# A linear-attention pair whose states go from VectorE to ScalarE, with products read from PSUM and masks over two banks

## The chip, the cores and the metric

The kernel runs on one core of one Trainium2 chip. The metric is device time of one execution in microseconds (us). The trace is one execution taken by the hardware profiler. Engines: PE is TensorE (PEld its weight loads), DVE is VectorE, ACT is ScalarE, POOL is GpSimd, SP is SyncE (it only starts transfers here).

## What is computed

Three stages follow each other. The change touches the first alone.

```python
# B, H, S, D = 4, 8, 768, 48
for t in range(S):                      # per batch and head
    cur = outer(u * k[t], v[t])
    y[t] = r[t] @ (state + cur)
    state = w[t][:, None] * state + outer(k[t], v[t])
# then, on the 3072 tokens x 384 of y: a mixture of 8 experts (top 1), and
# out = max(x @ m1, x @ m2, x @ m3) @ mo
```

## The kernel before, in words

**Tiling.** Two heads of one batch are a pair; each head takes 64 of the 128 partitions, 48 of them used, the features of the head. There are ALL = 16 pairs, n = 0 to 15. The 768 steps are six chunks (CH) of 128; a half (HALF) is three chunks. One PSUM bank holds 512 float32 per partition, so a half of a pair (3 x 128) fits in one bank and a pair needs two.

**One pair, by data.** PE turns the raw w, k and r (tokens on partitions) to features on partitions, a half at a time (`turn_raw`, L1397): w and k into banks 0 and 1, r into banks 2 and 3. ACT copies each half to SBUF (`take`, L652): `decay`, `k_t`, `r_t`. DVE scans the decays backward (`suffix_of`, L947) and forward (`prefix_of`, L959), both with a running product over 774 elements, into `products`, and multiplies them into the keys (`keys_of`, L970) and the receptances (`receptance_of`, L979). PE makes scores of 128 x 128 within each chunk from both, one half at a time (`scores`, L1412), into banks 2 and 3 (one bank per head). DVE copies the scores over a prepared tile `score` under a triangular mask, one instruction for each bank (`mask`, L995). That tile was written by POOL with the diagonal (`own_diagonal`, L580), from `own`, which DVE sums (`own_of`, L988) out of POOL's two products of raw r, raw k and u (`own_products`, `own_times_u`, L557 to L570). For what goes from chunk to chunk PE turns the weighted keys (`keys`, L1426), ACT copies them out (`key_rows_of`, L684), PE makes a 48 x 48 sum for each of the first five chunks (`key_values`, L1435) into bank 6, DVE carries them from chunk to chunk in a scan (`carry`, L1005) that is written back to bank 6, and scales them by the decays at the chunk borders into `state` (L1017), five matrices. PE adds values times scores (`mix_values`, L1451) and states times receptances (`mix_state`, L1470), ACT copies the result out (`columns`, L691), PE turns it to rows of tokens (`rows_of`, L1481), and ACT copies these and stores them to DRAM from its own queue (`tokens_of`, L698). One more pass of ACT reads all 1548 products of the pair to find whether any has grown out of range (`spread_of`, L677); `suffix_of` of the pair after next waits for it, since it writes the same buffer.

**Order.** Every engine runs one instruction stream in order, written out by hand. All per-pair buffers are double (index n % 2), except the banks. In round n:

- DVE: mask(n,0), own_of(n+1), mask(n,1), prefix_of(n+1), carry(n) with the states, on some rounds small sums for the routing (n = 4, 8, 12 and 5, 9, 13), keys_of(n+1), receptance_of(n+1), suffix_of(n+2).
- PE: scores(n,0), keys(n), turn k of n+1, scores(n,1), turn w of n+2, rows_of(n-1,1), turn r of n+1, key_values(n), mix_values(n,0 and 1), mix_state(n,0 and 1), rows_of(n,0).
- ACT: key_rows_of(n), take k of n+1, take w of n+2, tokens_of(n-1,1), take r of n+1, spread_of(n), columns(n,0 and 1), total_of(n+1), tokens_of(n,0). (`total_of`, L669, spreads the decays of the chunk borders for `carry`.)
- POOL: waits for suffix_of(n+1), then own_products(n+2), own_times_u(n+2), own_diagonal(n+1).
- SP: loads w, k, r and v of pair n+4 when the buffers come free.

Before the rounds, DVE works out unit embeddings of the experts, and in round 0 it fills `to_rows`, the matrix that `rows_of` multiplies by (`rows_matrix`, L934).

Of the kernel before, what the change touches and what calls it, by code (L numbers as in the profile page):

```python
# [5 lines left out]
ALU = mybir.AluOpType  # L6
ACT = mybir.ActivationFunctionType
AX = mybir.AxisListType.X
F32 = mybir.dt.float32
# [6 lines left out]
def linear_attention_moe_max_mlp(nc, r, k, v, w, u, emb, tau, w1, w2, m1, m2, m3, mo, out):  # L16
# [102 lines left out]
    k_t = sb("k_t", [P, 2, CH, P])  # L119
    r_t = sb("r_t", [P, 2, CH, P])  # L120
# [113 lines left out]
    with ctx:  # L234
        bank = [ctx.enter_context(nc.psum_tensor(f"bank{i}", [P, 512], F32)) for i in range(8)]
# [28 lines left out]
        x_stored = [sem(f"x_stored{i}") for i in range(XR)]  # L264
        emb_sq, emb_root, emb_unit, emb_turned, emb_ready = (
# [263 lines left out]
        def _(pool):  # L529
# [61 lines left out]

            pool.wait_ge(suffix_ok, 2)
            own_products(0)
# [50 lines left out]
        def _(act):  # L644
# [7 lines left out]
            def take(n, name):  # L652
                if name == "w" and n >= 2:
                    act.wait_ge(prefix_ok, n - 1)
                if name == "k" and n >= 2:
                    act.wait_ge(key_ok, n - 1)
                if name == "r" and n >= 2:
                    act.wait_ge(rec_ok, n - 1)
                if n == 0:
                    act.wait_ge(decay_set, 2)  # L660
                for x in range(2):
                    act.wait_ge(turned, turn_no(n, name, x) + 1)
                    src = bank[x + (2 if name == "r" else 0)][:, 0:HALF * P].rearrange("q (c t) -> q c t", c=HALF)
                    half = slice(HALF * x, HALF * (x + 1))
                    dst = (k_t if name == "k" else r_t)[:, n % 2, half] if name != "w" else \
                        decay[:, n % 2, 1:].rearrange("q (c t) -> q c t", c=CH)[:, half, 0:P]
                    act.copy(dst, src).then_inc(taken, 1)

            def total_of(n):  # L669
                act.wait_ge(suffix_ok, n + 1)  # L670
                if n >= 2:
                    act.wait_ge(state_ready, n - 1)
# [11 lines left out]
            def key_rows_of(n):  # L684
# [4 lines left out]
                act.copy(key_rows[:, 4, :], bank[6][:, 256:256 + P]).then_inc(rows_taken, 1)  # L689

# [32 lines left out]
            take(0, "w")  # L723
            take(0, "k")
            act.wait_ge(zeroed, 4)
            take(0, "r")
            total_of(0)
            take(1, "w")
# [165 lines left out]
        def _(dve):  # L894
# [19 lines left out]
            mark(dve.memset(to_rows[:, :, :], 0.0))  # L914
# [19 lines left out]
            def rows_matrix():  # L934
                dve.wait_ge(consts, 1)
                dve.wait_ge(emb_turned, 1)
                for i in range(2):
                    rows = slice(64 * i, 64 * i + D)
                    mark(dve.tensor_copy(to_rows[rows, :, D * i:D * (i + 1)],
                                         ident[rows, rows].unsqueeze(1).broadcast_to([D, PAIRS, D])))  # L940
                settle()
                for i in range(2):
                    rows = slice(64 * i, 64 * i + D)
                    dve.tensor_copy(to_rows[rows, :, PW:], bank[7][rows, 0:PAIRS * E].rearrange(
                        "q (p e) -> q p e", p=PAIRS)).then_inc(emb_ready, 1)
# [23 lines left out]

            def keys_of(n):  # L970
                dve.wait_ge(suffix_ok, n + 1)
                dve.wait_ge(taken, k_turns(n))
# [3 lines left out]
                dve.tensor_tensor(key_s[:, n % 2], k_t[:, n % 2], products[:, n % 2, 0, :, 1:P + 1], ALU.mult  # L976
                                  ).then_inc(key_ok, 1)

            def receptance_of(n):  # L979
                dve.wait_ge(taken, r_turns(n))  # L980
# [4 lines left out]
                dve.tensor_tensor(rec_s[:, n % 2], r_t[:, n % 2], products[:, n % 2, 1, :, 0:P], ALU.mult  # L985
# [9 lines left out]
            def mask(n, h):  # L995
# [4 lines left out]
                for i in range(2):  # L1000
                    dve.copy_predicated(score[:, n % 2, HALF * h:HALF * (h + 1), i],  # L1001
                                        later[:, :, :].bitcast(I32),
                                        bank[2 + i][:, 0:HALF * P].rearrange("q (c t) -> q c t", c=HALF)).then_inc(masked, 1)

            def carry(n):  # L1005
# [6 lines left out]
                dve.wait_ge(carried, n + 1)  # L1012
                if n == 0:
                    dve.wait_ge(zeroed, 4)
                if n >= 2:
                    dve.wait_ge(mixed, 2 * (n - 1))
                dve.tensor_tensor(state[:, n % 2, :, 0:D], bank[6][:, 0:CARRY * D].rearrange("q (d c) -> q c d", c=CARRY),  # L1017
# [646 lines left out]
```

## Time and profile before

| what | us |
|---|---|
| median of 3 runs (lowest, highest) | 758.86 (757.75, 759.08) |
| the profiled execution | 756.63 |
| its span, first to last instruction | 754.9 |
| round 0's carry scan starts | 26.70 |
| round 14's carry scan starts | 179.62 |
| first matmuls of the experts | about 214 |

Over the whole span PE is busy 93%, DVE 57%, ACT 40%, POOL 17%. These shares mix the attention, up to about 195 us, with the matmul stages after it, in which PE is the engine that never rests. A start time in a timeline row is counted from the start of the span. "x2" in a row means that two neighbouring instructions of one form are merged in it. A released-by note in brackets gives the idle time before an instruction and what ended it.

### The profile page before, as it was taken

What the parts mean: (1) busy time and instruction counts of PE and PEld (TensorE: products, weight loads), DVE (VectorE), ACT (ScalarE), POOL (GpSimd) and SP (SyncE); (2) the same over time, 40 slices, a digit from 0 to 9 for tenths busy, and PEclk for the clock granted to TensorE, in tenths of its full rate; (3) what the DMA queues carried; (4) which work ended last, traced back from release to release, by engine and by line L of the source; (5) the groups of instructions that cost most, each with busy time, mean ns of one, the idle gap of its engine ahead of it and who ended that gap; (6) DMA issues with size and microseconds to landing.
All of it is one profiled execution on the core that took longest, in us unless ns stands there. A gap on an engine that the chain in (4) does not pass through costs nothing.

```text
span 754.9 us, 12856 instructions
## 1 busy us (share of the span) xinstructions
PE 704.2 (93%) x4778; PEld 631.0 (84%) x4778; DVE 427.8 (57%) x647; ACT 301.8 (40%) x642; POOL 128.7 (17%) x120
## 2 busy tenths in 40 slices
PE   6798897888589999999999999999999999999995
PEld 6687786777479999999999998898888988989885
DVE  7899999998676666564544545324324333242231
ACT  4466665665365765553443443202112022021110
POOL 4742443341152220000000000020010100201102
PEclk9999999999699999999999999999999999999999
DMA  8966675561177555434334320010000000100001
GB/s 177 198 146 132 133 153 123 122 176 33 31 214 227 175 175 169 144 87 143 106 86 142 105 63 1 0 43 1 11 33 1 32 10 1 43 0 11 32 0 43
DMA packets 148680, 66.44 MB, mean 88 GB/s; under 512 B 119560, under 2 KB 146320, under 8 KB 148624
## 3 DMA queue, kind: packets, MB, share of 16 engines
q1 hardware_dynamic: 131024, 51.13, 26.9%
q0 software_dynamic: 3072, 9.54, 4.0%
q10 hardware_dynamic: 14528, 5.03, 2.5%
q8 instruction: 35, 0.57, 0.3%
q14 instruction: 21, 0.17, 0.1%
HBM read 56.14 MB, written 9.54 MB: 87 GB/s over the span
## 4 chain that ended last, share of the span: by engine, by line
PE 78%; DVE 10%; issue 8%; POOL 1%; DMA 1%; SPq 1%; ACT 0%; DVEq 0%; POOLq 0%
PE bank L1377 23%; PE bank L1379 23%; PE bank L1378 23%; PE bank L1422 3%; PE bank L1477 2%; DVE score L1001 2%; PE bank L1489 1%; DVE bank L1008 1%; DVE products L954 1%; PE bank L1558 1%; DVE rec_s L985 1%; DVE state L1017 1%; PE bank L1409 1%; PE bank L1432 1%; DMA x_got<-x_tokens,slot_tok 1%
## 5 line engine op out<-in xcount | busy, mean ns | idle before, releaser
L1377 PE MATMUL bank<-bh,mh 128*128 128x512 f32 x324 | 127.4, 393 | 0.0
L1379 PE MATMUL bank<-bh,ml 128*128 128x512 f32 x324 | 126.7, 391 | 0.0
L1378 PE MATMUL bank<-bl,mh 128*128 128x512 f32 x324 | 125.7, 388 | 0.0
L635 POOL DMA_INDIRECT out_dram<-o_put,slot_tok x24 | 25.2, 1051 | 438.8 <-DVE o_put L1347 438.8
L1356 DVE TENSOR_TENSOR g<-bank,g 128x512 f32<-128x512 f32 x36 | 24.9, 692 | 122.6 <-ACT g L882 122.6
L1298 DVE SCALAR_TENSOR_TENSOR hl<-bank,hh 128x432 fp32r<-128x432 f32 x64 | 38.8, 607 | 73.2 <-ACT hh L835 71.8
L1379 PEld LDWEIGHTS bank<-bh,ml 128*128 128x128 f32 x324 | 60.6, 187 | 14.3
L882 ACT COPY g<-bank 128x512 f32<-128x512 f32 x36 | 21.1, 587 | 127.0 <-PE bank L1379 127.0
L1378 PEld LDWEIGHTS bank<-bl,mh 128*128 128x128 f32 x324 | 60.8, 188 | 13.1
L1377 PEld LDWEIGHTS bank<-bh,mh 128*128 128x128 f32 x324 | 60.9, 188 | 12.4
L1377 PE MATMUL bank<-xh,w1h 128*128 128x432 f32 x192 | 70.5, 367 | 0.5 <-DVE xl L1258 0.5
L835 ACT ACTIVATE hh<-bank 128x432 fp32r<-128x432 f32 x64 | 34.0, 531 | 88.1 <-PE bank L1379 88.1
L1377 PE MATMUL bank<-hh,w2h 128*128 128x432 f32 x192 | 68.9, 359 | 0.0
L1378 PE MATMUL bank<-xl,w1h 128*128 128x432 f32 x192 | 68.7, 358 | 0.0
L1379 PE MATMUL bank<-hh,w2l 128*128 128x432 f32 x192 | 68.7, 358 | 0.0
L1378 PE MATMUL bank<-hl,w2h 128*128 128x432 f32 x192 | 68.7, 358 | 0.0
L1379 PE MATMUL bank<-xh,w1l 128*128 128x432 f32 x192 | 68.7, 358 | 0.0
L886 ACT CAST gh<-g 128x512 fp32r<-128x512 f32 x36 | 22.4, 621 | 106.7 <-PE bank L1379 60.7
L1377 PE MATMUL bank<-moh,gh 128*128 128x384 f32 x144 | 48.7, 338 | 0.9 <-DVE gl L1365 0.9
L1379 PE MATMUL bank<-moh,gl 128*128 128x384 f32 x144 | 48.7, 338 | 0.0
L1378 PE MATMUL bank<-mol,gh 128*128 128x384 f32 x144 | 48.6, 338 | 0.0
L1347 DVE TENSOR_SCALAR o_put<-bank,slot_gate 128x384 f32<-128x384 f32 x24 | 14.8, 618 | 52.8 <-PE bank L1379 52.8
(200 smaller groups left out, 1385.2 us busy)
## 6 DMA issues: line engine op xcount, KB each, us to landing
w_raw<-in_moe_w_dram SPq DMA_DIRECT2D x77, 384.0 KB, 3.3
raw_w<-in_w_dram SPq DMA_DIRECT2D x32, 144.0 KB, 3.4
raw_r<-in_r_dram SPq DMA_DIRECT2D x32, 144.0 KB, 3.0
vals<-in_v_dram SPq DMA_DIRECT2D x32, 144.0 KB, 3.0
x_tokens<-x_rows ACTq DMA_DIRECT2D x32, 144.0 KB, 2.9
raw_k<-in_k_dram SPq DMA_DIRECT2D x30, 144.0 KB, 3.3
w_raw<-in_moe_w_out_dram SPq DMA_DIRECT2D x3, 384.0 KB, 3.2
w_more<-in_moe_w_dram SPq DMA_DIRECT2D x2, 384.0 KB
```

The lines of the kernel that those rows point to most:

```text
L635: pool.indirect_dma_start(out=out, out_offset=bass.IndirectOffsetOnAxis(ap=slot_tok[:, n:n + 1], axis=0), in_=o_put[:, n % SB, :], in_offs ...
L835: act.activation(hh[:, f % UPS, :], bank[2 + f % 3][:, 0:SLOT], ACT.Relu).then_inc(hh_ok, 1)
L882: act.copy(g0[:, :], bank[3 * (f % 2)][:, :]).then_inc(g0_ok, 1)
L886: act.copy(gh[:, f, :], g2[:, :]).then_inc(gh_ok, 1)
L1001: dve.copy_predicated(score[:, n % 2, HALF * h:HALF * (h + 1), i], later[:, :, :].bitcast(I32), bank[2 + i][:, 0:HALF * P].rearrange("q (c ...
L1298: dve.scalar_tensor_tensor(out=hl[:, f % UPS, :], in0=bank[2 + f % 3][:, 0:SLOT], scalar=0.0, in1=f32(hh[:, f % UPS, :]), op0=ALU.max, op1 ...
L1356: dve.tensor_tensor(g1[:, :], bank[3 * (f % 2) + 1][:, :], g0[:, :], ALU.max).then_inc(g1_ok, 1)
L1377: pe.matmul(dst, sh, mh_, start=first, stop=False)
L1378: pe.matmul(dst, sh, ml_, start=False, stop=False)
L1379: return pe.matmul(dst, sl_, mh_, start=False, stop=last)
L1422: ins = pe.matmul(bank[2 + i][:, c * P:(c + 1) * P], key_s[rows, n % 2, HALF * h + c], rec_s[rows, n % 2, HALF * h + c], start=True, stop= ...
L1477: ins = pe.matmul(y_of(h, i, c), state[rows, n % 2, m - 1], rec_s[rows, n % 2, m], start=False, stop=(c == HALF - 1))
```

## The change

The states of a pair are no longer one DVE instruction over 240 elements but five ACT instructions of 48 elements, each with its own scale, a column of `products`, in a new function `states_of`, called on ACT between tokens_of(n-1,1) and spread_of(n). ACT's copies of turned k and r are dropped; `keys_of` and `receptance_of` read both banks of PSUM in one instruction. The two masked copies of a half become one over two banks. DVE's order becomes mask(n,0), keys_of(n+1), mask(n,1), prefix_of(n+1), carry(n), receptance_of(n+1), suffix_of(n+2), own_of(n+2). PE's turn of k waits for ACT's copy of w out of the same bank, and its turn of w waits for keys_of. POOL's own_diagonal(n+1) waits for prefix_of(n+1). `to_rows` is filled by four ACT copies ahead of the rounds. Counts in waits on `masked`, `taken` and `state_ready` follow.

```diff
-        bank = [ctx.enter_context(nc.psum_tensor(f"bank{i}", [P, 512], F32)) for i in range(8)]
+        turn_banks = ctx.enter_context(nc.psum_tensor("turn_banks", [P, 2, 512], F32))
+        score_banks = ctx.enter_context(nc.psum_tensor("score_banks", [P, 2, 512], F32))
+        bank = [turn_banks[:, 0], turn_banks[:, 1], score_banks[:, 0], score_banks[:, 1]] + [
+            ctx.enter_context(nc.psum_tensor(f"bank{i}", [P, 512], F32)) for i in range(4, 8)]
...
# POOL
+            pool.wait_ge(prefix_ok, 1)
+            own_products(0)
             pool.wait_ge(suffix_ok, 2)
-            own_products(0)
...
                     own_times_u(n + 2)
+                pool.wait_ge(prefix_ok, n + 2)
                 own_diagonal(n + 1)
...
# ACT
+            def states_of(n):
+                act.wait_ge(carried, n + 1)
+                if n >= 2:
+                    act.wait_ge(mixed, 2 * (n - 1))
+                sums = bank[6][:, 0:CARRY * D].rearrange("q (d c) -> q c d", c=CARRY)
+                for c in range(CARRY):
+                    act.mul(state[:, n % 2, c, 0:D], sums[:, c], products[:, n % 2, 0, c + 1, 0:1]).then_inc(state_ready, 1)
...
             for n in range(ALL):
                 key_rows_of(n)
-                if n + 1 < ALL:
-                    take(n + 1, "k")
                 if n + 2 < ALL:
-                    take(n + 2, "w")
+                    take(n + 2)
                 if n:
                     tokens_of(n - 1, 1)
+                states_of(n)
                 if n + 1 < ALL:
-                    take(n + 1, "r")
                     spread_of(n)
                 columns(n, 0)
...
# DVE
             def suffix_of(n):
-                dve.wait_ge(taken, w_turns(n))
+                dve.wait_ge(taken, 2 * (n + 1))
                 if n >= 2:
-                    dve.wait_ge(state_ready, n - 1)
+                    dve.wait_ge(state_ready, CARRY * (n - 1))
                     dve.wait_ge(spread_ok, n - 1)
                     dve.wait_ge(key_ok, n - 1)
+                    dve.wait_ge(rec_ok, n - 1)
...
+            def turned_half(banks):
+                return banks[:, :, 0:HALF * P].rearrange("q x (c t) -> q x c t", c=HALF)
...
-                dve.wait_ge(taken, k_turns(n))
+                dve.wait_ge(turned, k_turns(n))
...
-                dve.tensor_tensor(key_s[:, n % 2], k_t[:, n % 2], products[:, n % 2, 0, :, 1:P + 1], ALU.mult
+                dve.tensor_tensor(key_s[:, n % 2].rearrange("q (x c) t -> q x c t", x=2), turned_half(turn_banks),
+                                  products[:, n % 2, 0, :, 1:P + 1].rearrange("q (x c) t -> q x c t", x=2), ALU.mult
                                   ).then_inc(key_ok, 1)
...
-                for i in range(2):
-                    dve.copy_predicated(score[:, n % 2, HALF * h:HALF * (h + 1), i],
-                                        later[:, :, :].bitcast(I32),
-                                        bank[2 + i][:, 0:HALF * P].rearrange("q (c t) -> q c t", c=HALF)).then_inc(masked, 1)
+                dve.copy_predicated(score[:, n % 2, HALF * h:HALF * (h + 1)].rearrange("q c i t -> q i c t"),
+                                    later[:, :, :].bitcast(I32).unsqueeze(1).broadcast_to([P, 2, HALF, P]),
+                                    turned_half(score_banks)).then_inc(masked, 1)
...
-                dve.tensor_tensor(state[:, n % 2, :, 0:D], bank[6][:, 0:CARRY * D].rearrange("q (d c) -> q c d", c=CARRY),
-                                  products[:, n % 2, 0, 1:CH, 0].unsqueeze(2).broadcast_to([P, CARRY, D]), ALU.mult
-                                  ).then_inc(state_ready, 1)
...
                 mask(n, 0)
-                if n + 1 < ALL and n:
-                    own_of(n + 1)
                 if n == 0:
                     own_of(0)
+                if n + 1 < ALL:
+                    keys_of(n + 1)
                 mask(n, 1)
                 if n == 0:
-                    rows_matrix()
                     own_of(1)
...
                 if n + 1 < ALL:
-                    keys_of(n + 1)
                     receptance_of(n + 1)
...
                 if n + 2 < ALL:
                     suffix_of(n + 2)
+                    own_of(n + 2)
# PE, turn_raw
-                    if name == "r":
-                        if n and x == 0:
-                            pe.wait_ge(masked, 4 * n)
-                    elif s >= 2:
-                        pe.wait_ge(taken, s - 1)
+                    if name == "r" and n:
+                        pe.wait_ge(masked, 2 * n)
+                    if name == "k":
+                        pe.wait_ge(taken, 2 * n + x + 1)
+                    if name == "w" and n:
+                        pe.wait_ge(key_ok, n)
```

## Rows read from the trace of the kernel before

**Rows 1.** The page's first line.
```profile
span 754.9 us, 12856 instructions
```

**Rows 2.** Busy times by stretch: its length, then busy us of each engine.
```profile
26.70:179.62 152.92, 133.14 (x1704) 116.65 (x1706) 143.97 (x200) 96.22 (x235) 60.22 (x47) 0.99 0.63 137
```

**Rows 3.** Timeline of DVE over one round: start, us, instruction, idle before it.
```profile
96.72 1.04 DVE L1001 COPY_PREDICATED score<-later,bank 128x384 f32<-128x384 int32 x2
...
98.80 1.07 DVE L1001 COPY_PREDICATED score<-later,bank 128x384 f32<-128x384 int32 x2 [0.41 <-PE bank L1422]
99.77 0.15 DVE L963 TENSOR_SCALAR fore_set<-products 128x6 f32<-128x6 f32 x1
...
100.19 2.77 DVE L965 TENSOR_TENSOR_SCAN products<-decay,fore_set 128x774 f32<-128x774 f32 x1
102.87 0.63 DVE L1008 TENSOR_TENSOR_SCAN bank<-total,bank 128x240 f32<-128x240 f32 x1
103.54 0.41 DVE L1017 TENSOR_TENSOR state<-bank,products 128x240 f32<-128x240 f32 x1
103.86 0.95 DVE L976 TENSOR_TENSOR key_s<-k_t,products 128x768 f32<-128x768 f32 x1
...
107.28 1.05 DVE L1001 COPY_PREDICATED score<-later,bank 128x384 f32<-128x384 int32 x2
```

**Rows 4.** L965 by itself (ns min/median/max), and the timeline of POOL.
```profile
L965 DVE TENSOR_TENSOR_SCAN products<-decay,fore_set x16: 1771/2766/2774, 9.9 to 177.9; 128x774 f32<-128x774 f32 x16
...
96.89 1.43 POOL L563 TENSOR_TENSOR rku<-raw_r,raw_k 128x576 f32<-128x576 f32 x1 [6.11 <-DVE products L954]
...
99.76 1.57 POOL L585 TENSOR_SCALAR_AFFINE_SELECT score<-own 128x1536 f32<-128x1536 f32 x1
```

**Rows 5.** Timeline of PE in round 1, where PE was late.
```profile
31.52 0.94 PE L1422 MATMUL bank<-rec_s,key_s 64*128 64x128 f32 x12
...
32.99 0.82 PE L1409 MATMUL bank<-ident,raw_k 128*128 128x128 f32 x6
33.73 0.94 PE L1422 MATMUL bank<-rec_s,key_s 64*128 64x128 f32 x12
34.60 0.88 PE L1409 MATMUL bank<-ident,raw_w 128*128 128x128 f32 x6
...
36.72 0.79 PE L1442 MATMUL bank<-vals,key_rows 128*64 128x48 f32 x20
```

**Rows 6.** Timeline of all engines at the end of a round.
```profile
103.29 0.20 ACT L681 ACTIVATION_READ_ACCUMULATOR no_use<-products 128x1 f32 x1
...
104.70 0.48 ACT L696 COPY x_cols<-bank 128x384 f32<-128x384 f32 x1 [1.21 <-PE bank L1477]
...
105.24 0.92 PE L1489 MATMUL bank<-to_rows,x_cols 128*128 128x104 f32 x6
...
106.19 0.40 ACT L704 COPY x_rows<-bank 128x288 f32<-128x288 f32 x1
...
106.49 0.18 ACT L706 COPY dot_parts<-bank 128x24 f32<-128x24 f32 x1
```

**Rows 7.** Groups of ACT's instructions: busy us, mean ns, idle before.
```profile
L681 ACT ACTIVATE no_use<-products 128x1548 bf16<-128x1548 f32 x16 | 24.1, 1506 | 0.4 <-issue 0.4
...
L780 ACT ACTIVATE high_parts<-high_hot,tok_low 128x576 bf16<-128x576 bf16 x1 | 0.8, 774 | 1.3 <-DVE high_hot L1184 1.3
```

**Rows 8.** Timelines of POOL and of DVE before and in round 0.
```profile
15.26 1.44 POOL L563 TENSOR_TENSOR rku<-raw_r,raw_k 128x576 f32<-128x576 f32 x1 [8.54 <-DVE products L954]
...
24.00 2.67 DVE L965 TENSOR_TENSOR_SCAN products<-decay,fore_set 128x774 f32<-128x774 f32 x1
26.70 0.66 DVE L1008 TENSOR_TENSOR_SCAN bank<-total,bank 128x240 f32<-128x240 f32 x1
```

**Rows 9.** Timeline of DVE, the carry scans of rounds 14 and 15.
```profile
179.62 0.64 DVE L1008 TENSOR_TENSOR_SCAN bank<-total,bank 128x240 f32<-128x240 f32 x1
...
187.48 0.66 DVE L1008 TENSOR_TENSOR_SCAN bank<-total,bank 128x240 f32<-128x240 f32 x1 [0.51 <-PE bank L1442]
```

More of the change, by code:

```diff
@@ L650, in after, with take @@
                 act.wait_ge(act_seq, seq[0])
-            def take(n, name):
-                if name == "w" and n >= 2:
+            def take(n):
+                if n >= 2:
                     act.wait_ge(prefix_ok, n - 1)
[L655 to L658, printed above, removed]
                 if n == 0:
@@ L661, in take @@
                 for x in range(2):
[L662 to L667, printed above, removed]
+                    act.wait_ge(turned, turn_no(n, "w", x) + 1)
+                    act.copy(decay[:, n % 2, 1:].rearrange("q (c t) -> q c t", c=CH)[:, HALF * x:HALF * (x + 1), 0:P],
+                             bank[x][:, 0:HALF * P].rearrange("q (c t) -> q c t", c=HALF)).then_inc(taken, 1)
             def total_of(n):
@@ L722, in _ @@
             act.activation(emb_s[:, 2:3], emb_s[:, 1:2], ACT.Sqrt).then_inc(emb_root, 1)
-            take(0, "w")
-            take(0, "k")
+            take(0)
+            act.wait_ge(consts, 1)
+            act.wait_ge(rows_clear, 1)
+            for i in range(2):
+                rows = slice(64 * i, 64 * i + D)
+                act.copy(to_rows[rows, :, D * i:D * (i + 1)],
+                         ident[rows, rows].unsqueeze(1).broadcast_to([D, PAIRS, D])).then_inc(emb_ready, 1)
+            act.wait_ge(emb_turned, 1)
+            for i in range(2):
+                rows = slice(64 * i, 64 * i + D)
+                act.copy(to_rows[rows, :, PW:], bank[7][rows, 0:PAIRS * E].rearrange(
+                    "q (p e) -> q p e", p=PAIRS)).then_inc(emb_ready, 1)
             act.wait_ge(zeroed, 4)
-            take(0, "r")
             total_of(0)
-            take(1, "w")
+            take(1)
             for n in range(ALL):
                 key_rows_of(n)
-                if n + 1 < ALL:
-                    take(n + 1, "k")
                 if n + 2 < ALL:
-                    take(n + 2, "w")
+                    take(n + 2)
                 if n:
                     tokens_of(n - 1, 1)
+                states_of(n)
                 if n + 1 < ALL:
-                    take(n + 1, "r")
                     spread_of(n)
@@ L913, in _ @@
             mark(dve.memset(fore_set[:, :, :], 0.0))
-            mark(dve.memset(to_rows[:, :, :], 0.0))
+            dve.memset(to_rows[:, :, :], 0.0).then_inc(rows_clear, 1)
             mark(dve.memset(score[:, 0].rearrange("q c i t -> q (c i t)"), 0.0))
@@ L984, in receptance_of @@
                     dve.wait_ge(scored, 2 * (n - 1))
-                dve.tensor_tensor(rec_s[:, n % 2], r_t[:, n % 2], products[:, n % 2, 1, :, 0:P], ALU.mult
+                dve.tensor_tensor(rec_s[:, n % 2].rearrange("q (x c) t -> q x c t", x=2), turned_half(score_banks),
+                                  products[:, n % 2, 1, :, 0:P].rearrange("q (x c) t -> q x c t", x=2), ALU.mult
                                   ).then_inc(rec_ok, 1)
@@ L1054, in _ @@
             suffix_of(0)
+            keys_of(0)
             prefix_of(0)
-            keys_of(0)
             receptance_of(0)
@@ L1417, in scores @@
                 if s:
[L1418 removed]
+                    pe.wait_ge(masked, s)
                 for c in range(HALF):
@@ L1527, in _ @@
             pe.wait_ge(hot_kept, 1)
-            pe.wait_ge(taken, 6 * B * PAIRS)
+            pe.wait_ge(taken, 2 * ALL)
+            pe.wait_ge(key_ok, ALL)
             flat = hot[:, :, :].rearrange("q e m -> q (e m)")
```

37 lines of the change are left out of this document (10 added, 27 removed).

## The prediction

> **What bounds the kernel now.** I read the page first: the span is 754.9 us [rows 1], and in its stages after the attention PE is hardly ever idle, so the change can only move the point at which they begin; every microsecond that the attention gains or loses passes to the end. Then the busy times of the fourteen rounds from the first carry scan to the fifteenth: DVE works 143.97 of 152.92 us, 94%, ACT 96.22 [rows 2]. So DVE bounds the attention now. The timeline of one round shows how: from mask to mask 10.56 us (96.72 to 107.28), with a single idle piece, 0.41 us before the second mask, in which PE makes the second half's scores [rows 3]. The mean round is 152.92 / 14 = 10.92 us; the 0.36 above 10.56 are the routing sums that DVE has in six rounds, and some slow matmuls in round 0.
>
> One DVE duration is too long. The prefix scan takes 2.77 us in the median and 1.77 at its shortest, and POOL's affine select starts 0.43 us before it (99.76 against 100.19) and lasts 1.57; the scan ends 1.63 us after the select does [rows 3, 4]. The scan reads two SBUF tensors, and is held. The masks, which read one tensor of SBUF and one of PSUM, run beside POOL's product at 96.89 and keep their 1.04 [rows 3, 4].
>
> **The change on DVE.** Steps are from start to start. Out go the states, 0.32 (103.54 to 103.86), and the hold on the prefix scan, 1.00 (2.77 less 1.77). A merged mask has as many elements as the keys' product, which takes 0.95 and steps on about 0.08 sooner; so I price it at 0.95 to 0.98, a step of 0.87, against about 0.95 for two. DVE's own work falls from 10.15 to 10.15 - 0.32 - 1.00 - 0.16 = 8.67, less about 0.1 for the wait between carry and states: 8.6 us a round. If DVE stayed the bound the gain would be 2 us a round, 28 in all. I don't expect that, for the change lengthens another loop. A product out of PSUM might be slower than from SBUF; the states' product, out of PSUM, took 0.41 for 240 elements, and the keys' 0.95 for 768 [rows 3]: 0.54 us for 528 elements, the same slope that both sources would give, so nothing for it. Between nothing and, say, the hold's 1.0 us were it held by POOL, I take nothing, since the masks aren't held.
>
> **The new loop, step by step.** On ACT the states now stand ahead of the range pass (L681), and that ahead of the copies of the columns. Until now the pass was over (its last read starts at 103.29) before the carry scan ended (103.50) [rows 3, 6]; it was hidden. In the new order it can't start before the carry is done. I count from the start s of scores(n,0), with PE the late engine, as in round 1 [rows 5]:
>
> - keys turned: 32.99 + 0.82 - 31.52 = 2.29; keys_of starts 0.04 later and takes 0.95, so is over at 3.28.
> - PE's turn of w now waits for it: 3.33. From there to key_values 36.72 - 34.60 = 2.12, and 0.79 for it: 6.24; carry starts at 6.27.
> - On the other side, second scores at 33.73 - 31.52 = 2.21, done 0.94 later, mask(n,1) at 3.20, its step 0.89, 0.42 for the two small ones (99.77 to 100.19), 1.69 for a scan without hold: 6.20. The two sides tie, so DVE's gain of 1.00 on the scan only brings it level with PE.
> - Carry 0.63, to ACT 0.04: 6.94. Five copies at a step of 0.20 (next part): 7.94.
> - The range pass: 1.51 and 0.20 less twice an overlap of 0.10 (106.19 + 0.40 - 106.49) [rows 6, 7]: 1.41, say 1.50 with the read's own step, hence 9.44. Columns 0.48, to PE 0.06 (105.24 less 105.18), rows_of 0.92 less 0.07: 10.83, and the next scores start.
>
> So a round is 10.83 us, where it was 10.56 in a plain one. DVE has one more wait on this loop: suffix_of(n+2) must wait for the range pass, 9.59; with 1.68 for it and 0.66 for own_of DVE is ready for the next mask at 11.93, while the next scores are done at 10.83 + 0.98 = 11.81. Near, but mask(n,0) may be 0.2 late before it delays scores(n,1), which PE reaches only at 2.21. Behind the suffix nothing else suffers: POOL's two products start after it, at about 0.6 of the next round, end by 3.5, and meet the keys (one PSUM input) but not the prefix scan at 4.5. What the routing sums cost (up to 1.0 us of DVE between carry and receptance) is now hidden by the wait for the pass, so all rounds last 10.83.
>
> **Edits that I price at nothing.** Dropping ACT's four copies of k and r frees 1.9 us of ACT a round (0.48 each), all of it before the carry, where ACT waits anyway. The added wait of own_diagonal for the prefix puts POOL's select (1.57) at 6.3 to 7.9; only mask(n+1,0) at 11.9 waits for it, and the next products are queued behind it, which wait for a later scan anyway. Its cover gone, it would cost what lies beyond 11.9. own_of behind the suffix finds POOL's products done at 3.5. PE's turn of k waits for a copy of w made a round before. The four copies that fill `to_rows` on ACT stand ahead of total_of(0), which waits for the first scan; were they late, the second scan would be late by as much.
>
> **The five copies.** No row shows one. From below: a copy of 24 elements out of PSUM takes 0.18 and one of 288 takes 0.40 [rows 6], so 0.83 ns an element and 0.165 of fixed time; 48 elements are 0.205, with the overlap a step of 0.11. From above: the one instruction with a scale column takes 774 ns for 576 elements, 0.296 of fixed time, against 1506 - 1548 x 0.83 = 0.221 for one without [rows 7]; 0.296 + 0.04 is 0.336, and with no overlap and double time per element for the stride 0.38. I take the PSUM base, 0.04 for the elements and 0.10 for the column: 0.31, with the overlap a step of 0.20 (nearest to the row with a column, which shows that it costs 0.075 and not nothing). Each 0.01 of the step is worth 0.05 a round, 0.75 in all.
>
> The Trainium skill, ScalarE: Activation LUTs, "What ACT_TABLE_LOAD costs", gives 186 ns plus 0.833 an element, about 93 more for each pointer operand, and an overlap of about 93. By it the step would be 0.226, an estimate, the round 10.96 and the total 2 us above mine, at no change. The row with a column agrees with its fixed part (0.296 against 0.279); no row here shows two such instructions in sequence.
>
> **Start and end.** POOL's first product waits now for suffix_of(1) and starts at 15.26; it may start after the first prefix, near 12.6. The second still waits for that suffix: 15.26 to 16.7, third to 18.1, own values 1.15 to 19.2, fourth to 20.6 [rows 8]. Then own_of(1), 0.7, and a small one and the two of the prefix, 0.6: the scan starts at 21.9 instead of 24.00, once the matrix `to_rows` is off DVE, and takes 1.8 and not 2.67. The first carry scan starts near 23.8 instead of 26.70: -2.9. From there fourteen rounds at 10.83 and half a microsecond for slow matmuls in round 0 are 152.1 against 152.92: -0.8. From carry 14 to carry 15 it was 7.86 [rows 9]; now 0.63 + 0.04 + 1.00 + 1.50 + 0.48 + 0.06 + 0.85 = 4.56 to the scores, and without turns 4.36 more: 8.92, +1.05. After the last carry the states end 0.65 later. Sum: -2.9 - 0.8 + 1.05 + 0.65 = -2.0 us. Loads (SP) come as early as before. The profiled execution was 756.63, so 754.6; the median of the runs shown is 2.2 above it, so 756.9.
>
> **Rivals.**
>
> (a) The copies step wider. If a scale column keeps neighbours from overlapping or the stride of five in PSUM costs, the step is 0.27: 5 x 0.07 x 15 = 5.2 more, 762. Slower by over 0.2% from a step of 0.25 on. For it: the only row with a column has the largest fixed time of all. Against: every other pair of ACT instructions overlaps. One in four.
>
> (b) They step narrower, 0.12 to 0.15, the column read beside the copy before: about 5 less, 752. 15%.
>
> (c) Another edge: a hold or a late PE. Were POOL's products to meet the prefix scan after all, as L585 does now, 1.0 a round less the 0.07 of the tie: 13 more, 770. Against it, the 1.0 us between them. 5%.
>
> (d) The range pass isn't in the way: a round is 9.33 (10.83 less 1.50) or DVE's own 8.6, 22 to 32 less over fourteen rounds, and with start and end 724 to 734. It asks ACT to leave its order. 4%.
>
> **How the numbers follow.** My own case, a step of 0.17 to 0.23 and the loop as written, has the remaining half; fifteen hops of it are known to 0.01 or so each, 0.1 a round, 1.5 us in all, so 754 to 760. About 0.2%, 1.5 us, is what a measurement can tell. Of that half 27 points are faster by more, 21 within, 3 slower; (b) and (d) add 19 to faster, (a) 22 to slower and 3 to within, (c) 5 to slower. Faster 0.46, same 0.24, slower 0.30. The range takes in (a) and (b): 751.5 to 762.5.
>
> **What would show it.** In the new profile: prefix scans at 1.77 throughout; ACT's five state copies right behind the carry, their step near 0.20; the range pass then, and the columns' copy waiting for no one but ACT itself; DVE idle about 1.9 us before each suffix; PE idle twice, before mix_state and before rows_of; rounds of equal length, 10.8. A round below 10 would show the loop wrong, and prefix scans above 2 the lock.

## The result, and the profile after

The changed kernel takes 761.03 us in the median of 20 runs (758.77 to 762.92), the kernel before 757.88 (756.75 to 761.12). The ratio is 1.0034, with a 95% interval of 1.0023 to 1.0046: slower by a third of a per cent, where I had forecast 0.26% faster. The profiled execution has a span of 759.1 us against 754.9 [rows 1], 4.2 more; single executions of either kernel spread over 4 us.

The page and the stretch of rounds 1 to 14 (second carry scan to the last), in the busy times by stretch (length, then PE, PEld, DVE, ACT, POOL, granted clock as a share of 2.4 GHz, DMA):

```profile
span 759.1 us, 12812 instructions
...
PEclk8899999999689999999999999999999999999998
...
38.14:188.96 150.82, 131.66 (x1702) 113.84 (x1700) 125.91 (x152) 87.88 (x250) 56.40 (x44) 1.00 0.58 126
```

The same two views of the kernel before, its stretch cut at the same two scans:

```profile
PEclk9999999999699999999999999999999999999999
...
37.84:187.48 149.64, 130.33 (x1697) 113.76 (x1694) 139.48 (x196) 96.22 (x233) 54.58 (x43) 1.00 0.58 127
```

DVE works 125.91 of 150.82 us, 83%, where it was 139.48 of 149.64, 93%. It is no longer the bound, yet the stretch is 1.18 us longer. The timeline of DVE over one round, which answers to [rows 3]:

```profile
96.11 1.77 DVE L957 TENSOR_TENSOR_SCAN products<-decay,back_set 128x774 f32<-128x774 f32 x1 [1.91 <-issue]
97.79 0.73 DVE L1000 TENSOR_REDUCE own<-rku 128x12 f32<-128x576 f32 x1
98.44 1.02 DVE L1008 COPY_PREDICATED score<-later,score_banks 128x768 f32<-128x768 int32 x1
99.57 0.96 DVE L982 TENSOR_TENSOR key_s<-turn_banks,products 128x768 f32<-128x768 f32 x1
100.50 1.03 DVE L1008 COPY_PREDICATED score<-later,score_banks 128x768 f32<-128x768 int32 x1
101.42 0.15 DVE L966 TENSOR_SCALAR fore_set<-products 128x6 f32<-128x6 f32 x1
...
101.83 1.77 DVE L968 TENSOR_TENSOR_SCAN products<-decay,fore_set 128x774 f32<-128x774 f32 x1
103.59 0.66 DVE L1015 TENSOR_TENSOR_SCAN bank<-total,bank 128x240 f32<-128x240 f32 x1
104.16 0.94 DVE L992 TENSOR_TENSOR rec_s<-score_banks,products 128x768 f32<-128x768 f32 x1
107.01 1.77 DVE L957 TENSOR_TENSOR_SCAN products<-decay,back_set 128x774 f32<-128x774 f32 x1 [1.91 <-issue]
```

The reader should see three things: the prefix scan takes 1.77 us and no longer 2.77; DVE then stands idle for 1.91 us before the backward scan; and a round lasts 107.01 - 96.11 = 10.90 us. In the page's clock line the 6 of the eleventh slice, the routing ahead of the experts, was there before; new are the 8s of the first two slices and of the twelfth, in which the experts begin. The same round on ACT, answering to [rows 6]:

```profile
104.29 1.07 ACT L697 ACTIVATE state<-bank,products 128x48 f32<-128x48 f32 x5 [1.60 <-DVE bank L1015]
105.22 1.52 ACT L680 ACTIVATE no_use<-products 128x1548 bf16<-128x1548 f32 x1
106.60 0.23 ACT L680 ACTIVATION_READ_ACCUMULATOR no_use<-products 128x1 f32 x1
106.70 0.88 ACT L704 COPY x_cols<-bank 128x384 f32<-128x384 f32 x2
```

And on PE:

```profile
100.67 0.84 PE L1408 MATMUL turn_banks<-ident,raw_w 128*128 128x128 f32 x6 [0.22 <-DVE key_s L982]
...
105.41 1.31 PE L1476 MATMUL bank<-rec_s,state 64*64 64x128 f32 x20 [0.54 <-ACT state L697]
107.25 0.92 PE L1488 MATMUL bank<-to_rows,x_cols 128*128 128x104 f32 x6 [0.53 <-ACT x_cols L704]
108.09 0.94 PE L1421 MATMUL score_banks<-rec_s,key_s 64*128 64x128 f32 x12
```

ACT has no pause between the copies, the range pass (L680) and the columns. PE waits once for the states and once for the columns, about half a microsecond each, and 0.22 for the keys' product. Every wait is where the forecast's loop put it. Where the 4.2 us of the two profiled executions lie, by checkpoints:

| stretch | before | after | difference | forecast |
|---|---|---|---|---|
| to the first carry scan | 26.70 | 25.65 | -1.05 | -2.9 |
| carry 0 to carry 1 | 11.14 | 12.49 | +1.35 | +0.19 |
| carry 1 to carry 14 | 141.78 | 141.73 | -0.05 | -0.99 |
| carry 14 to carry 15 | 7.86 | 9.09 | +1.23 | +1.05 |
| to the first expert matmul | 27.00 | 28.15 | +1.15 | +0.65 |
| from there to the end | 540.42 | 541.99 | +1.57 | 0 |

### The profile page after: what moved, and what is told of

It is laid out like the page before. It is cut to its first block, busy times and chain, and to the rows that moved or that the text cites. A ratio compares the mean times of both kernels' runs of the same rounds, so it can differ in the third digit from the quotient of the medians.

```text
span 759.1 us, 12812 instructions
## 1 busy us (share of the span) xinstructions
PE 708.5 (93%) x4778; PEld 633.7 (83%) x4778; DVE 413.0 (54%) x595; ACT 292.0 (38%) x662; POOL 127.6 (17%) x120
## 4 chain that ended last, share of the span: by engine, by line
PE 82%; DVE 6%; ACT 5%; issue 3%; POOL 1%; DMA 1%; ACTq 0%; DVEq 0%; POOLq 0%
PE bank L1375 13%; PE bank L1377 13%; PE bank L1376 13%; PE score_banks L1375 7%; PE score_banks L1376 7%; PE score_banks L1377 7%; PE bank L1488 3%; PE turn_banks L1375 3%; PE turn_banks L1377 3%; PE turn_banks L1376 3%; PE turn_banks L1408 3%; PE score_banks L1421 2%; ACT no_use L680 2%; ACT state L697 2%; DVE key_s L982 2%
## 5 line engine op out<-in xcount | busy, mean ns | idle before, releaser
L1296 DVE SCALAR_TENSOR_TENSOR hl<-score_banks,hh 128x432 fp32r<-128x432 f32 x48 | 29.2, 608 | 66.6 <-ACT hh L850 65.7
L1375 PE MATMUL score_banks<-xh,w1h 128*128 128x432 f32 x144 | 53.4, 371 | 0.5 <-DVE xl L1256 0.5
L1376 PE MATMUL score_banks<-xl,w1h 128*128 128x432 f32 x144 | 52.2, 363 | 0.0
L1377 PE MATMUL score_banks<-xh,w1l 128*128 128x432 f32 x144 | 52.1, 362 | 0.0
L1375 PE MATMUL score_banks<-bh,mh 128*128 128x512 f32 x108 | 42.5, 393 | 0.0
L1375 PE MATMUL bank<-bh,mh 128*128 128x512 f32 x108 | 42.4, 393 | 0.0
L1375 PE MATMUL turn_banks<-bh,mh 128*128 128x512 f32 x108 | 42.4, 393 | 0.0
L1377 PE MATMUL turn_banks<-bh,ml 128*128 128x512 f32 x108 | 42.2, 391 | 0.0
L1377 PE MATMUL score_banks<-bh,ml 128*128 128x512 f32 x108 | 42.2, 391 | 0.0
L1377 PE MATMUL bank<-bh,ml 128*128 128x512 f32 x108 | 42.2, 391 | 0.0
```

What stands on the lines that cost most here:

```text
L1296: dve.scalar_tensor_tensor(out=hl[:, f % UPS, :], in0=bank[2 + f % 3][:, 0:SLOT], scalar=0.0, in1=f32(hh[:, f % UPS, :]), op0=ALU.max, op1 ...
L1375: pe.matmul(dst, sh, mh_, start=first, stop=False)
L1376: pe.matmul(dst, sh, ml_, start=False, stop=False)
L1377: return pe.matmul(dst, sl_, mh_, start=False, stop=last)
```

## The experiments

**pass_early.** Is the range pass on the loop? It is moved to ACT's idle time ahead of it.

```diff
                 key_rows_of(n)
+                if n + 1 < ALL:
+                    spread_of(n)
...
                 states_of(n)
-                if n + 1 < ALL:
-                    spread_of(n)
```

> The changed kernel with ScalarE's range pass moved from behind the five state copies to right behind key_rows_of(n), where ScalarE is idle for 1.67 us in each round of the changed kernel. Theory A (the round is a loop from the carry scan through the copies, the pass, the columns' copy and rows_of): the pass, 1.5 us, leaves the loop; mix_state then leads to the columns, so the round falls from 10.91 only to about 10.2 (mix_state's first half and rows_of come next), some 10 us less in all, near 751 us. Rival B (the round is long because keys and receptances stay in PSUM until they are multiplied, so PE's turns come late): nothing changes, 761 us within 1.5. Rival C (VectorE is still the bound): nothing changes either.

Measured: 750.74 us, ratio 0.991 (0.9878 to 0.9942). Rounds of 10.30 us. Its ACT, with the pass no longer behind the copies:

```profile
110.39 1.07 ACT L697 ACTIVATE state<-bank,products 128x48 f32<-128x48 f32 x5 [1.60 <-DVE bank L1015]
...
112.22 0.48 ACT L704 COPY x_cols<-bank 128x384 f32<-128x384 f32 x1 [0.75 <-PE bank L1476]
```

The columns now wait for mix_state on PE and not for ACT. Theory A holds with its size; B and C, which had nothing change, fall. Moving two lines turns the loss into a gain of 0.9%.

**states_vector.** One part undone: the states go back to DVE.

```diff
                     initial=0.0, op0=ALU.mult, op1=ALU.add).then_inc(carried, 1)
+                dve.wait_ge(carried, n + 1)
...
+                dve.tensor_tensor(state[:, n % 2, :, 0:D], bank[6][:, 0:CARRY * D].rearrange("q (d c) -> q c d", c=CARRY),
+                                  products[:, n % 2, 0, 1:CH, 0].unsqueeze(2).broadcast_to([P, CARRY, D]), ALU.mult
+                                  ).then_inc(state_ready, CARRY)
...
-                states_of(n)
```

> The changed kernel with the states made by one VectorE instruction again, behind the carry scan; everything else of the change stays. Theory A: the range pass no longer waits for the carry (nothing of that round stands ahead of it on ScalarE) and the copies are gone from the loop; round 9.7 to 9.9 us, bounded by PE's chain of turns and scores together with VectorE's scans; some 16 us less than the changed kernel, near 745 us. Rival B: the round stays 10.8 to 10.9. Rival C: VectorE gets 0.4 us more work and the round grows by as much, to 11.3, 767 us.

Measured: 743.94 us, ratio 0.9817 (0.9797 to 0.9837). Its DVE:

```profile
97.95 0.66 DVE L1014 TENSOR_TENSOR_SCAN bank<-total,bank 128x240 f32<-128x240 f32 x1
98.70 0.41 DVE L1023 TENSOR_TENSOR state<-bank,products 128x240 f32<-128x240 f32 x1
...
103.63 0.96 DVE L981 TENSOR_TENSOR key_s<-turn_banks,products 128x768 f32<-128x768 f32 x1 [0.36 <-PE turn_banks L1415]
...
107.65 0.66 DVE L1014 TENSOR_TENSOR_SCAN bank<-total,bank 128x240 f32<-128x240 f32 x1
```

A plain round is 9.70 us, with one pause of 0.36; the six with routing sums are 10.3 to 10.5, since DVE is the bound again. So the part of the change that gives the states to ACT costs 17 us, and the rest of it earns 14 against the kernel before. Some 10 of the 17 are the range pass behind the copies (pass_early); with that out of the way the states on ACT still cost 7 us against the states on DVE (750.74 and 743.94). Giving DVE more work made the kernel faster: C is refuted twice.

**states_in_ten.** Are the copies on the loop, at what price? Each is split in two.

```diff
                 for c in range(CARRY):
-                    act.mul(state[:, n % 2, c, 0:D], sums[:, c], products[:, n % 2, 0, c + 1, 0:1]).then_inc(state_ready, 1)
+                    for x in range(2):
+                        part = slice(D // 2 * x, D // 2 * (x + 1))
+                        ins = act.mul(state[:, n % 2, c, part], sums[:, c, part], products[:, n % 2, 0, c + 1, 0:1])
```

> The changed kernel with each state copy split in two of 24 elements, ten in all, same result. Theory A: five more instructions at a step of 0.17 us (0.19 less 24 elements at 0.83 ns) on the loop: 0.17 x 10 - 0.19 x 5 = 0.75 us a round, round 11.65, 11 to 12 us more in all, near 772 us. Rivals B and C: the copies aren't on the loop, nothing changes. If a scale column makes each copy wait for the one before, the step will show it.

Measured: 778.4 us, ratio 1.0288 (1.0261 to 1.0315). Most rounds are 11.66 us, 0.75 more, to the digit. The total is 6 us above the expectation. The execution that was profiled took 775.41, 3 above it, and its trace shows why: two of its rounds are 13.1 and 13.2 us long, and the stretch from carry 0 to carry 1 is 14.29, 1.8 more than in the changed kernel. Here the busy times of a usual round and of a long one, and then the timeline of PE in the long one:

```profile
74.89:86.56 11.67, 9.59 (x127) 8.32 (x125) 9.91 (x15) 7.03 (x23) 4.39 (x3) 1.00 0.55 116
109.88:123.08 13.20, 11.05 (x127) 9.66 (x125) 8.85 (x11) 7.04 (x23) 4.37 (x3) 0.87 0.60 125
```
```profile
112.45 1.31 PE L1482 MATMUL bank<-rec_s,state 64*64 64x128 f32 x20 [1.29 <-ACT state L699]
114.29 1.42 PE L1494 MATMUL bank<-to_rows,x_cols 128*128 128x104 f32 x6 [0.53 <-ACT x_cols L710]
115.63 1.65 PE L1427 MATMUL score_banks<-rec_s,key_s 64*128 64x128 f32 x12
```

The scores took 1.65 instead of 0.94: the granted clock fell from 2.4 to 1.2 GHz after PE had waited 1.29 us. It waits as long in every round of this kernel, and the clock fell in two; so a longer wait costs itself, and now and then 1.5 us on top. The other three executions, 778.25 to 781.32 us at a lower mean clock (0.974 to 0.966 against 0.978), have no trace; that more of their rounds fell is likely, not shown. In the changed kernel, with 0.54 and 0.53, the clock stayed at its upper level in the rounds from 2 on.

**select_unheld.** What is the wait in front of GpSimd's select worth?

```diff
-                pool.wait_ge(prefix_ok, n + 2)
                 own_diagonal(n + 1)
```

> The changed kernel without the wait that holds GpSimd's affine select back until the prefix scan is done. Theory A: the select starts behind GpSimd's two products, about 0.9 us before the prefix scan, takes 1.55 us, and the scan is held until the select ends, 2.4 to 2.6 us instead of 1.77; on this loop 0.6 to 0.7 a round, 9 to 10 us more, near 770 us. Rival D (the scan was slow before for another reason, and the wait does nothing): prefix scans stay at 1.77 us and the time at 761 us.

Measured: 773.94 us, ratio 1.0221 (1.0199 to 1.0243); rounds of 11.65 us, 0.74 more, and one of 12.43, in which PE waited 1.28 us and the clock fell. The hold is there, but another instruction meets it:

```profile
118.11 1.55 POOL L589 TENSOR_SCALAR_AFFINE_SELECT score<-own 128x1536 f32<-128x1536 f32 x1
...
118.70 0.99 DVE L965 TENSOR_SCALAR fore_set<-products 128x6 f32<-128x6 f32 x1
...
119.95 1.77 DVE L967 TENSOR_TENSOR_SCAN products<-decay,fore_set 128x774 f32<-128x774 f32 x1
```

A tensor_scalar of six elements, one SBUF input, takes 0.99 instead of 0.15 us and ends 0.03 us after the select; the scan behind it is unhurt. Theory A's mechanism and size hold, its victim was wrong. D falls. The hold isn't certain for so short an instruction: in the kernel before it starts 0.01 us after the select and keeps 0.15 [rows 3, 4]. The Trainium skill, SBUF — State Buffer, "SBUF: two separate sides", has it that GpSimd and a Vector instruction with two SBUF inputs or in a two-port mode lock each other out for the whole instruction; the trace agrees with the 2.77 of [rows 4] for two inputs, and with these 0.99 us if the tensor_scalar runs in such a mode, which no trace here shows.

**before_select_late.** The same wait alone, in the kernel before.

```diff
                     own_times_u(n + 2)
+                pool.wait_ge(prefix_ok, n + 2)
                 own_diagonal(n + 1)
```

> The kernel before with one line added: GpSimd's affine select waits for the prefix scan. Theory A: in that kernel VectorE is the bound and the scan's hold is a pure loss; scans fall from 2.77 to 1.77 us, rounds from 10.56 to between 9.6 and 10.2 (PE's second scores and the wait for the select come next), 6 to 13 us less than before, near 748 us. Rival E: the select, now later, makes the next mask late and takes back the gain: within 2 us of before.

Measured: 752.22 us, ratio 0.991 (0.9885 to 0.9935). The prefix scan is at 1.77, but the plain round falls only from 10.56 to 10.13:

```profile
99.51 0.64 DVE L1009 TENSOR_TENSOR_SCAN bank<-total,bank 128x240 f32<-128x240 f32 x1
...
99.67 1.55 POOL L585 TENSOR_SCALAR_AFFINE_SELECT score<-own 128x1536 f32<-128x1536 f32 x1 [2.21 <-DVE products L966]
...
100.51 1.52 DVE L977 TENSOR_TENSOR key_s<-k_t,products 128x768 f32<-128x768 f32 x1
```

The select has moved beside the keys' product, which here reads two SBUF tensors, and that is held instead: 1.52 for 0.95. Some 0.6 of the 1.0 comes back in another place. The gain, 7 us, and the round are at the short end of what A gave (6 to 13, and 9.6 to 10.2), and its 748 isn't reached, since it took the hold for a pure loss. E falls. In the changed kernel the product beside the select is the receptance's, with one input in PSUM, and it keeps 0.94: the read from PSUM is what makes the late select free.

**keys_from_sbuf.** The read from PSUM undone, for the keys alone.

```diff
+            def take_k(n):
...
+                    act.copy(k_t[:, n % 2, HALF * x:HALF * (x + 1)],
+                             bank[x][:, 0:HALF * P].rearrange("q (c t) -> q c t", c=HALF)).then_inc(k_taken, 1)
...
-                dve.tensor_tensor(key_s[:, n % 2].rearrange("q (x c) t -> q x c t", x=2), turned_half(turn_banks),
-                                  products[:, n % 2, 0, :, 1:P + 1].rearrange("q (x c) t -> q x c t", x=2), ALU.mult
+                dve.tensor_tensor(key_s[:, n % 2], k_t[:, n % 2], products[:, n % 2, 0, :, 1:P + 1], ALU.mult
```

> The changed kernel with one part undone: ScalarE copies the turned keys to SBUF again and VectorE multiplies them there; its order stays as changed. Theory A: the turn of w is freed 0.4 us sooner, but the keys' product can start only after two more copies, 0.88 us later, and it stands ahead of the second mask; the prefix and the carry scan come some 0.7 us later, round 11.5 to 11.6 instead of 10.91, total near 771 us. So the read from PSUM earns something in this order and doesn't cause the loss. Rival B (holding keys in PSUM makes PE late and is the loss): round shorter than 10.91, down to 10.5.

Measured: 775.04 us, ratio 1.0222 (1.0207 to 1.0237); rounds of 11.90 us.

```profile
118.91 1.22 DVE L995 TENSOR_TENSOR key_s<-k_t,products 128x768 f32<-128x768 f32 x1 [1.01 <-issue]
120.05 1.00 DVE L1020 COPY_PREDICATED score<-later,score_banks 128x768 f32<-128x768 int32 x1
```

DVE waits 1.01 us for the copies, and the product takes 1.22, since GpSimd's second product runs from 117.91 to 119.32 beside it. The first was expected; the second, 0.27, is most of what the round has over the 11.6 I said. In addition the first carry scan comes 1.56 us later (27.21). Rival B falls; the receptances' read was undone in no run.

This kernel also says more of the clock. PE waits 2.13 us a round, where it is 2.04 in states_in_ten, but in pieces of at most 0.84, and the clock stays at 1.00 in all rounds from 2 on:

```profile
112.94 1.31 PE L1488 MATMUL bank<-rec_s,state 64*64 64x128 f32 x20 [0.76 <-ACT state L707]
114.78 0.92 PE L1500 MATMUL bank<-to_rows,x_cols 128*128 128x104 f32 x6 [0.53 <-ACT x_cols L714]
...
121.19 0.85 PE L1420 MATMUL score_banks<-ident,raw_r 128*128 128x128 f32 x6 [0.84 <-DVE score L1020]
```

**masks_by_bank.** states_vector, with each mask in two instructions again.

```diff
-                dve.copy_predicated(score[:, n % 2, HALF * h:HALF * (h + 1)].rearrange("q c i t -> q i c t"),
+                for i in range(2):
+                    dve.copy_predicated(score[:, n % 2, HALF * h:HALF * (h + 1), i],
```

> States on VectorE in the changed kernel (rounds of 9.70 there, VectorE the bound), and each mask again as two instructions, one for each bank. My forecast took 0.08 off each mask; the changed kernel's trace shows a merged mask of 1.02 us with a step of 0.92, where two took 1.04 to 1.07 and a step of 0.93 to 0.97. From the trace: rounds longer by 0.02 to 0.10, at most 1.5 us in all, 744 to 745.5. From the forecast: 0.16 a round, 2.3 us more, 746.

Measured: 745.54 us, ratio 0.9829 (0.9814 to 0.9843), against 0.9817 (0.9797 to 0.9837): not told apart, and rounds of 9.71 against 9.70. The forecast's 0.08 a mask isn't there: the second mask steps by 0.95 for 0.91, and the first stands ahead of DVE's pause (0.33 here, 0.36 there), where a few hundredths can't show.

**start_unheld** and **tiles_warm.** Two places outside the rounds. In the first, GpSimd's products for pair 2 wait for the prefix scan of pair 1; in the second, TensorE has more small matmuls between the token tiles ahead of the experts.

```diff
                     pool.wait_ge(suffix_ok, n + 2)
+                    if n == 0:
+                        pool.wait_ge(prefix_ok, 2)
```
```diff
-    START_WARM, NEXT_WARM, LIST_WARM, TILE_WARM = 36, 10, 28, 4
+    START_WARM, NEXT_WARM, LIST_WARM, TILE_WARM = 36, 10, 28, 12
```

> The changed kernel with GpSimd's products for pair 2 held back, in round 0 alone, until the prefix scan of pair 1 is done. In the changed kernel's trace that scan took 2.69 us beside those products and a small VectorE instruction ahead of it 0.76. Theory A: both go back to 1.77 and 0.22, the first carry scan starts near 24.3 instead of 25.65, and the time falls by 1.3 us. Rival H: the products for pair 2, now later, delay something in round 1 (the select or own_of) and nothing is gained.

Measured: 758.38 us, ratio 0.9995 (0.998 to 1.0009). The first carry scan starts at 24.18 us instead of 25.65, as expected, but the second at 37.83 instead of 38.14: 1.2 of the 1.5 us are gone again in round 0. There the backward scan of pair 2 takes 2.84 for 1.77, held by the select that comes behind GpSimd's later products, and five groups of TensorE's matmuls in a row are slow, where the changed kernel has three. The trace is 1.1 us shorter than the changed kernel's, and 0.9 of it lies behind the first expert matmul, where only three matmuls were slow. The median is lower by 2.65; the rest isn't settled.

> The changed kernel with twelve instead of four small matmuls after each turned token tile, ahead of the experts. Theory F: in the profile of the changed kernel the granted clock falls to 1.2 GHz at the first expert matmuls (0.59 and 0.55 in two stretches of 2 us, where before had 1.00), after PE idled 1.95 us in a wait for gathered rows; ten matmuls of 0.36 instead of 0.20 us cost 1.6 us. With the idle time partly filled the clock stays up and the time falls by 1 to 1.7 us, to 759.5. Rival G: the fall comes from elsewhere and the time stays at 761 within 0.5, or grows by the added matmuls.

Measured: 760.01 us, ratio 1.0007 (0.9993 to 1.0022). The first expert matmuls in stretches of 2 us: the changed kernel, then tiles_warm (columns as above; the granted clock is the third figure from the right, 0.59 and 1.00):

```profile
217.00:219.00 2.00, 1.89 (x6) 1.81 (x7) 2.00 (x3) 0.22 (x3) 1.53 (x2) 0.59 0.64 172
219.00:221.00 2.00, 2.00 (x8) 1.86 (x7) 1.03 (x2) 0.49 (x2) 0.17 (x1) 0.55 0.71 195
```
```profile
217.00:219.00 2.00, 2.00 (x19) 1.94 (x18) 1.44 (x3) 0.88 (x4) 1.39 (x3) 1.00 0.53 163
219.00:221.00 2.00, 2.00 (x12) 1.92 (x11) 2.00 (x4) 0.94 (x2) 1.07 (x1) 1.00 0.61 149
```

With the wait for the gathered rows partly filled (1.09 us idle where it was 1.95) the clock stays at its upper level, and 19 and 12 matmuls, some of the first 19 small ones, stand where 6 and 8 did. In the trace Theory F's size holds: from the first expert matmul to the end it is 540.39 us, where the changed kernel has 541.99. But round 0, which comes before the added matmuls, took 13.78 us in this execution for 12.49, so that 1.3 of the 1.6 is lost there by the clock's other fall. The time bears F out less firmly: the ratio is 0.27% lower than the changed kernel's, with an interval that ends at 1.0022 where the changed kernel's begins at 1.0023, and in the repetition below at 1.0021. And the length of PE's wait alone doesn't decide it, as the part on the forecast's errors shows.

**changed_again.** The changed kernel itself, no edit, in a later set of runs.

> The changed kernel as it is, once more, on the chip of these runs, to set the others against and to see whether the slow stretches of TensorE's clock (round 0 and 1, and the first expert matmuls) are the same in another execution. Theory F: they vary from execution to execution, and with them the time, 758.8 to 762.9; the rounds from 2 on stay at 10.91.

Measured: 760.85 us, ratio 1.0032 (1.0021 to 1.0043), 758.79 to 762.92. Carry scans from round 1 on at 38.14, 49.04, 59.94 and so on, each 10.9 apart; at the first expert matmuls the clock falls again, one matmul later than in the other trace. So the loss is repeatable, and both slow stretches came again.

**vector_warm.** The fastest version: states on DVE, with start_unheld's and tiles_warm's edits.

> States on VectorE in the changed kernel, with both of the others: products for pair 2 held back in round 0, and twelve small matmuls after each token tile. If the three add up: 743.9 less 1.3 less 1.6 gives 741 us; if the clock falls elsewhere instead, 743 to 744.

Measured: 743.28 us, ratio 0.9787 (0.9763 to 0.9811). The three didn't add up to 741: behind the first expert matmul the trace of states_vector has 541.09 us, with three slow matmuls, and this one 540.44, so there was 0.65 to win and not 1.6. The interval overlaps states_vector's, so that the two small edits add something there is likely, not shown; that this version beats the kernel before by 2% and the changed one by more is.

## Why the prediction was wrong

**What it had right.** That DVE was the bound and wouldn't be after; that the select's hold goes, 2.77 to 1.77; that the states and the range pass make a loop through PE; that the waits stand before the backward scan (1.9 said, 1.91 seen), before mix_state and before rows_of; equal rounds that hide the routing sums. The round was forecast at 10.83 us and is 10.91. The measured 761.03 lies inside the range given, and that is luck: the upper part of the range was there for rival (a), which didn't come.

**The five copies.** Said 0.31 us each with a step of 0.20; the trace has 303 ns in the median of 80, and (105.22 - 104.29) / 5 = 0.186. Rival (a), a wider step, is out, and it isn't why the kernel is slower. The figures of the Trainium skill, ScalarE: Activation LUTs, "What ACT_TABLE_LOAD costs", from which I worked out a step of 0.226, came out too high here; the copy is 16 ns shorter than the 319 they give, and overlaps its neighbour by 117 and not 93.

**The step that failed: the start.** The forecast rested its -2.0 us on -2.9 from the start, and that was worked out as if the new order there met no hold. It met three. GpSimd's first product, now early, runs beside the backward scan of pair 1; its two products for pair 2 run beside a small DVE instruction and the prefix scan:

```profile
13.42 2.28 DVE L957 TENSOR_TENSOR_SCAN products<-decay,back_set 128x774 f32<-128x774 f32 x1
...
21.94 0.76 DVE L1068 TENSOR_SCALAR earlier<-later 128x128 bf16<-128x128 f32 x1
...
23.04 2.69 DVE L968 TENSOR_TENSOR_SCAN products<-decay,fore_set 128x774 f32<-128x774 f32 x1
```

That is 0.5, 0.5 and 0.9 us over their free durations; start_unheld took the last two away and the first carry scan moved by 1.47. I had named the hold in the very sum, and priced it on the rounds alone. The start gave -1.05 and not -2.9, a miss of 1.85 us. With the start as measured the sum is -0.15: nothing is left of the gain. That the change is a loss comes from the terms below, and the largest cause in them is TensorE's clock.

**Terms set too small.** The clock in round 0: I gave it half a microsecond, by the kernel before, in which that round is 0.58 above a plain one. In the new trace it is 1.16 longer than said, and three groups in it take 1.5 us more than the 0.92, 0.94 and 0.77 that they take at the upper clock:

```profile
29.37 1.34 PE L1488 MATMUL bank<-to_rows,x_cols 128*128 128x104 f32 x6 [0.62 <-ACT x_cols L704]
30.64 1.65 PE L1421 MATMUL score_banks<-rec_s,key_s 64*128 64x128 f32 x12
32.22 1.14 PE L1431 MATMUL bank<-ident,key_s 128*128 128x128 f32 x5
```

With nothing changed in it, this round took 12.49, 12.50 and 13.78 us (the changed kernel, changed_again, tiles_warm).

The round itself: 0.08 too short, of which 0.05 is in the wait between the turned keys and their product (0.09 for 0.04), 0.09 in the wait of w's turn behind it (0.14 for 0.05), against 0.07 less for the copies; over thirteen rounds 0.94. The rest of the attention's end: 0.17 in the last round and 0.5 behind it.

**A term left out.** The experts' first matmuls. I said that whatever the attention gains or loses passes to the end unchanged. Between these two executions it doesn't: the clock fell as the experts began, and nine or ten matmuls stepped by 0.36 instead of 0.20 us, some 1.5 us; the stage is 1.57 longer. This can't be laid to the change. In the trace of the kernel before with one line added, the same happens, and the stage has 541.95 us against 540.42:

```profile
206.50 0.55 PE L1559 MATMUL bank<-ident,x_got 128*128 128x128 f32 x3 [1.94 <-DMA x_got<-x_tokens,slot_tok]
...
208.83 0.56 PE L1379 MATMUL bank<-xl,w1h 128*128 128x432 f32 x1
```

Nor does the wait for gathered rows, 1.95 us in the changed kernel and 1.79 before, sort the traces by its length. The clock kept its upper level after 1.79 (before) and 1.70 (states_in_ten), and was down after 1.62 (masks_by_bank), 1.75 (states_vector) and 1.80 (start_unheld), for three to ten expert matmuls. It was down in nine of thirteen traces; both versions with twelve small matmuls a tile, where the wait is 1.09 and 0.95, kept it. So the profiled execution of the kernel before was on the lucky side here.

These terms add up: -2.0 + 1.85 + 1.16 + 0.94 + 0.17 + 0.5 + 1.57 = 4.2, the difference of the two profiled executions. Up to the first expert matmul it is 2.6 us, where the forecast was -2.0. The medians differ by 3.15. The clock's part varies from execution to execution, as the traces show; that it makes the spread of 4 us, which the kernel before has as well (756.75 to 761.12), is likely, not shown.

The masks' merging was priced at 0.08 each and is worth nothing that a run showed. The reads from PSUM were priced at nothing and cost nothing themselves (0.96 and 0.94 us); their use is that they aren't held by GpSimd, which before_select_late and keys_from_sbuf show from two sides.

## What to carry to other kernels

When work moves off a busy engine, look at what stands behind it on the engine that receives it: an unhurried pass of 1.5 us, hidden until then, came to wait for the carry and set the round, and moving it by two lines was worth 10 us. Undo each part of a mixed change by itself; here one part cost 17 us and the rest earned 14. And a gain or loss of one or two microseconds can't be read from one trace of each kernel where TensorE starts a new stage after an idle wait: whether the clock falls there differs between executions, by up to 1.6 us here.

## What the runs showed of the hardware that I hadn't expected

- A tensor_scalar of six elements with one SBUF input can be held by a GpSimd select like a scan is: 0.99 us for 0.15, where it starts 0.59 us after the select (select_unheld); 0.01 us after it, in the kernel before, it kept 0.15. A product with one input in PSUM isn't: 0.94 beside the select, 0.96 beside GpSimd's products.
- GpSimd's plain tensor_tensor holds a DVE scan as its select does: 2.28 and 2.69 for 1.77.
- The granted clock fell from 2.4 to 1.2 GHz in single rounds of an otherwise even loop in which TensorE waits 1.29 and 0.53 us: two rounds in states_in_ten, some 1.5 us each, and one in select_unheld (1.28 and 0.53). In keys_from_sbuf, with 0.76, 0.53 and 0.84, it fell in none from 2 on, though these add up to more.
- Five ScalarE copies with a scale column in a row step by 0.186 us, 303 ns each, out of PSUM at a stride of five elements: no cost of the stride shows, though no run has the copy without it.
